# The order of the attention items on five engines: one schedule table for another

## The chip, the cores and the metric

The kernel runs on one core of a Trainium2 chip. The metric is the device time of one execution in microseconds. Each engine (TensorE, VectorE, ScalarE, GpSimd, and SyncE, which issues all DMAs) runs its own list of instructions in order; they meet only in semaphores.

## The reference

Three layers follow each other. The first is a gated linear attention with complex gates, over batch 4, 8 heads, sequence 768, head size 48:

```python
mag = np.sqrt(a_re * a_re + a_im * a_im)
scale = np.minimum(mag, 0.999) / (mag + 1e-06)
a_re_n, a_im_n = (a_re * scale, a_im * scale)
for t in range(S):
    new_re = ar * S_re - ai * S_im
    new_im = ar * S_im + ai * S_re
    S_re, S_im = (new_re + kv, new_im)      # kv: outer product of k[t] and v[t]
    y[:, :, t] = np.einsum('bhd,bhde->bhe', q[:, :, t], S_re)
```

Its output, as 3072 rows of 384, goes through two feed-forward layers: `elu(x @ w_in) @ w_out` with 2048 hidden columns, and `max(x @ w1, x @ w2, x @ w3) @ w_out` with 768. Everything is fp32.

## The kernel before

**Tiling.** The sequence is cut into 6 chunks of 128 steps. A unit is one chunk of two of the four batches, so there are 12 units (u) and 24 items (n = 2u and 2u+1, called "a" and "b" in the tables). Within a chunk the recurrence is done in parallel: log magnitude and angle of the gates are summed along time by scans, q and k are multiplied with the decays and rotated, sent through DRAM to be transposed, and then TensorE makes scores and outputs.

**The gate chain of a part** (part 0 and 1 are the two halves of unit 0, part p is unit p-1 from 2 on; a part has 384 columns in the first two and 768 after). ScalarE `square` (L709), GpSimd or VectorE `square_im`, VectorE `squared` (L968), ScalarE `root` (L716), VectorE `denominator` (L974) and `negative`, ScalarE `small` (L726, three operations) and `inverse` (L735, two), `tangent` on GpSimd (VectorE in the first two parts), ScalarE `arctan` (L742, with a table load before and after), VectorE `log_decay`, `signed`, `angle`, `scan_lam`, `center`, `scan_phi`, `reduced` (L984 to L1048), ScalarE `exps` (L751) and `end_gains` (called ends), GpSimd `decayed` (L607, twice), ScalarE `sines` (L767, with table loads), VectorE `rotate_q` and `rotate_k` (L1050, L1062).

**The items of a batch n.** SyncE `store_q`, `store_k`, then `load_qt`, `load_kt` bring the turned q and k back transposed. TensorE: `scores(n)` (here s(n), 16 matmuls from kt and qt), `k_rows(n)` (kr(n), 8 transposes), `outputs(n)` (y(n)), `increment(n)` (inc(n)). VectorE: `masked(n)` copies the scores out of PSUM under the mask, `state_decayed(n)` multiplies the state, `state_add(n)` adds the increment, `x_low(n)` makes the low part of the layer's output; ScalarE: `k_rows` and `x_high(n)`. These TensorE results live in a ring of 3 PSUM banks (L363 to L390); the order in which the banks are taken is the order of the table, and a bank is refilled only after its last reader.

**The first feed-forward layer** runs beside the attention, in 96 groups g. TensorE `first(g)` (L1310) and `second(g)` (L1329), two groups behind; ScalarE `exp_g` and `high_g` (expg, highg), VectorE `elu_g` (elu), GpSimd `low_g` (lowg). first(g) needs elu(g-2), second(g) needs lowg(g), expg(g) needs first(g) and lowg(g-2). first(0) needs the output of batch 1, first(8) that of batch 3, first(16) that of batch 7. fp32 products are made of three fp32r matmuls with high and low parts; the parts of the weights are made by `w_in_high`, `w_out_high` (ScalarE), `w_in_low` (VectorE), `w_out_low` (GpSimd, here wolow). The last layer runs alone on the engines from about 600 us.

**What sets the order.** Every item has a position x. For unit u it is 16u plus the entry of a table: AT_FIRST for u = 0 (AT_FIRST_B for part 1), AT_SECOND for u = 1, AT for the rest (L55 to L99). SPLIT (L100) holds the positions of the weights' loads and splits. Each engine's function `attention(x)` runs, for rising x, those items that have this x, in the fixed sequence of its own `if` lines (L507, L648, L847, L1145, L1350). Positions below START = 16 are run ahead of group 0; the others are spread between the halves of the groups by `after` (L337): one position per half group from g = 16 on. SyncE has no groups and only runs through x. So a table entry does nothing by itself: two items change places on an engine only if their entries cross.

Of the kernel before, what the change touches and what calls it, by code (L numbers as in the profile page):

```python
# [18 lines left out]
def build(nc, q, k, v, a_re, a_im, w_in, w_out, w1, w2, w3, w_fin, out):  # L19
# [46 lines left out]

    AT_FIRST = {
        "square": -49, "square_im": -49, "squared": -48, "root": -43, "denominator": -43, "inverse": -41, "log_decay": -39,
        "signed": -36, "tangent": -40, "arctan": -38, "angle": -35, "scan_lam": -39, "center": -38, "exps": -35, "ends": -28,
        "scan_phi": -35, "reduced": -34, "decayed_a": -33, "decayed_b": -32, "sines": -31, "rotate_q_a": -28, "rotate_k_a": -26,  # L70
        "rotate_q_b": -26, "rotate_k_b": -23, "state_decay": -13, "s_a": -5, "s_b": 1, "kr_a": -3, "kr_b": 2, "masked_a": -2,
        "masked_b": 2, "kr_evac_a": -1, "kr_evac_b": 3, "state_decayed_a": -22, "state_decayed_b": -12, "y_a": -1, "y_b": 3,
        "inc_a": 0, "inc_b": 3, "state_add_a": -1, "state_add_b": 6, "x_high_a": 0, "x_low_a": -1, "x_high_b": 4, "x_low_b": 6,
        "load_a": -50, "load_q": -48, "load_k": -44, "load_v": -44, "store_q_a": -27, "load_qt_a": -24, "store_k_a": -26,
        "load_kt_a": -24, "store_q_b": -24, "load_qt_b": -23, "store_k_b": -24, "load_kt_b": -20, "store_ends": -21,
        "load_ends": -12, "tile": -2, "negative": -41, "small": -41,
    }
# [7 lines left out]
    AT_SECOND = {
        "square": -40, "square_im": -38, "squared": -40, "root": -36, "denominator": -35, "inverse": -30, "log_decay": -29,
        "signed": -27, "tangent": -28, "arctan": -29, "angle": -23, "scan_lam": -28, "center": -24, "exps": -27, "ends": -28,
        "scan_phi": -22, "reduced": -18, "decayed_a": -28, "decayed_b": -27, "sines": -16, "rotate_q_a": -13, "rotate_k_a": -12,
        "rotate_q_b": -2, "rotate_k_b": -7, "state_decay": 8, "s_a": 1, "s_b": 6, "kr_a": 3, "kr_b": 10, "masked_a": 0,
        "masked_b": 7, "kr_evac_a": 2, "kr_evac_b": 8, "state_decayed_a": 5, "state_decayed_b": 5, "y_a": 3, "y_b": 10,  # L90
        "inc_a": 3, "inc_b": 11, "state_add_a": 3, "state_add_b": 11, "x_high_a": 3, "x_low_a": 3, "x_high_b": 11,
        "x_low_b": 11, "load_a": -62, "load_q": -60, "load_k": -59, "load_v": -2, "store_q_a": -15, "load_qt_a": -6,
        "store_k_a": -7, "load_kt_a": -5, "store_q_b": 1, "load_qt_b": 5, "store_k_b": 2, "load_kt_b": 5, "store_ends": -23,
        "load_ends": -19, "tile": 14, "negative": -34, "small": -30,
    }
# [1370 lines left out]
```

How the kernel before makes its waits and increments, by code:

```python
        def of_gate(eng, first, later, p):  # L306
            if p < PAIR:
                eng.wait_ge(first, p + 1)
            else:
                eng.wait_ge(later, p - 1)
# [1 line left out]
        def of_rows(eng, z):  # L312
            if z < 2 * PAIR:
                eng.wait_ge(qkd1, z + 1)
            else:
                eng.wait_ge(qkd, z - 2 * PAIR + 1)
# [1 line left out]
        def gates_loaded(eng, p):  # L319
            u = unit_of_part(p)
            if u == 0:
                eng.wait_ge(l_first[p], 32)
            else:
                eng.wait_ge(l_a[u % 2], 32 * ((u + 1) // 2))
# [52 lines left out]
        def filling(pe, what, n):  # L377
            z = place[what, n]
            if z >= RING:
                pe.wait_ge(free[z % RING], z // RING)
            return bank[ATT + z % RING], full[z % RING]
# [1 line left out]
        def filled(eng, what, n):  # L383
            z = place[what, n]
            eng.wait_ge(full[z % RING], z // RING + 1)
            return bank[ATT + z % RING], free[z % RING]
# [1 line left out]
        def emptied(eng, what, n):  # L388
            z = place[what, n]
            eng.wait_ge(free[z % RING], z // RING + 1)
# [36 lines left out]
            def load_a(p):  # L427
                u = unit_of_part(p)
                if users(p):
                    sp.wait_ge(phi0, users(p))
                if u == 0:
                    sp.dma_start(gates(p).ar, a_re[0, :, p:p + 1, :]).then_inc(l_first[p], 16)
                    sp.dma_start(gates(p).ai, a_im[0, :, p:p + 1, :]).then_inc(l_first[p], 16)
# [191 lines left out]
            def low_g(g):  # L625
                pool.wait_ge(ghi, g + 1)
                if g >= GR:
```

## Time and profile before

| | us |
|---|---|
| median of 3 runs | 900.1 |
| lowest and highest | 899.71 and 901.69 |
| the profiled execution | 900.1 |
| its span, first to last instruction | 898.3 |

| engine | busy us | share of the span | instructions |
|---|---|---|---|
| TensorE (PE) | 834.2 | 93% | 5584 |
| VectorE (DVE) | 425.3 | 47% | 628 |
| ScalarE (ACT) | 488.2 | 54% | 731 |
| GpSimd (POOL) | 318.1 | 35% | 254 |

The mean granted TensorE clock is 0.992 of full speed. The chain of work that ended last is 85% TensorE by the profile. The shares are means over stages; single stretches differ from them.

### The profile page before, as it was taken

Reading aid. Unit: us, or ns where it says so; the run is one execution under the profiler, and the core shown is the slowest. Engines: PE = TensorE matmul, PEld = TensorE weight load, DVE = VectorE, ACT = ScalarE, POOL = GpSimd, SP = SyncE. Lnnn points to the kernel's source line nnn. Section 1 sums busy time; section 2 is a strip of 40 time slices with the busy share of each in tenths; the row PEclk is TensorE's granted clock in tenths of the full one; section 3 lists DMA queues with packets and bytes.
Section 4 is the critical chain, followed back from the end, with each engine's and each line's share of the span. In section 5 each row is a group of like instructions: output and inputs, shape, how many; then the busy total and the mean of one; then the engine's idle time right before and its main releaser. Section 6 shows DMA issues by size and latency. Waiting matters only on the chain.

```text
span 898.3 us, 14185 instructions
## 1 busy us (share of the span) xinstructions
PE 834.2 (93%) x5584; PEld 712.9 (79%) x5584; DVE 425.3 (47%) x628; ACT 488.2 (54%) x731; POOL 318.1 (35%) x254
## 2 busy tenths in 40 slices
PE   0168989899999999999999999999999999999998
PEld 0158979888888888888888888888888888888886
DVE  6679795857475747574757422333112121202120
ACT  7778778586868686868686535643121121112111
POOL 1064643534343434343434323555122131313021
PEclk9998999999999999999999999999999999999999
DMA  7684353453435352534352533011010202000000
GB/s 301 167 220 127 94 177 92 144 159 111 140 93 161 108 144 90 165 104 134 100 168 66 161 119 147 0 49 75 13 59 0 71 1 71 0 36 1 24 13 35
DMA packets 70146, 88.43 MB, mean 98 GB/s; under 512 B 15296, under 2 KB 52672, under 8 KB 69568
## 3 DMA queue, kind: packets, MB, share of 16 engines
q1 hardware_dynamic: 70080, 87.53, 31.8%
q8 instruction: 44, 0.72, 0.4%
q14 instruction: 22, 0.18, 0.1%
HBM read 59.13 MB, written 28.39 MB: 97 GB/s over the span
## 4 chain that ended last, share of the span: by engine, by line
PE 85%; issue 4%; ACT 4%; POOL 3%; DVE 3%; DMA 1%; SPq 0%; DVEq 0%; ACTq 0%; POOLq 0%
PE bank L1243 83%; ACT t L704 2%; POOL gl L593 1%; PE bank L1258 1%; DMA ai<-in_a_im 1%; DVE t L944 1%; POOL wol L593 1%; POOL t L590 1%; DVE t L947 1%; DVE sc L947 0%; ACT L707 0%; ACT cs L704 0%; ACT woh L704 0%; ACT sn L704 0%; ACT xh L704 0%
## 5 line engine op out<-in xcount | busy, mean ns | idle before, releaser
L593 POOL TENSOR_TENSOR gl<-ge,gh 128x512 fp32r<-128x512 f32 x96 | 131.5, 1373 | 246.1 <-ACT gh L704 246.1
L947 DVE TENSOR_TENSOR hm<-bank,hm 128x512 f32<-128x512 f32 x72 | 49.8, 692 | 225.0 <-PE bank L1243 223.2
L1243 PE MATMUL bank<-gh,woh 128*128 128x512 f32 (+1 forms) x336 | 125.1, 372 | 1.2 <-POOL gl L593 1.2
L1243 PE MATMUL bank<-xh,wah 128*128 128x512 f32 x324 | 126.0, 389 | 0.0
L1243 PE MATMUL bank<-xl,wah 128*128 128x512 f32 x324 | 126.0, 389 | 0.0
L1243 PE MATMUL bank<-xh,wal 128*128 128x512 f32 x324 | 126.0, 389 | 0.0
L1243 PE MATMUL bank<-xh,wih 128*128 128x512 f32 (+1 forms) x336 | 123.5, 368 | 2.6 <-DVE ge L944 1.3
L1243 PE MATMUL bank<-xh,wil 128*128 128x512 f32 (+1 forms) x336 | 121.2, 361 | 0.0
L1243 PE MATMUL bank<-xl,wih 128*128 128x512 f32 (+1 forms) x336 | 121.1, 361 | 0.0
L1243 PE MATMUL bank<-gl,woh 128*128 128x512 f32 (+1 forms) x336 | 121.0, 360 | 0.0
L1243 PE MATMUL bank<-gh,wol 128*128 128x512 f32 (+1 forms) x336 | 120.9, 360 | 0.0
L593 POOL TENSOR_TENSOR hl<-hm,hh 128x512 fp32r<-128x512 f32 x36 | 46.5, 1292 | 204.3 <-ACT hh L704 204.3
L944 DVE SCALAR_TENSOR_TENSOR ge<-ge,bank 128x512 f32<-128x512 f32 x96 | 65.8, 686 | 104.8 <-ACT ge L704 104.0
L704 ACT ACTIVATE ge<-bank 128x512 f32<-128x512 f32 x96 | 57.0, 594 | 85.5 <-PE bank L1243 82.5
L704 ACT ACTIVATE t<-t 128x768 f32<-128x768 f32 (+1 forms) x117 | 91.8, 790 | 10.7 <-DVE t L947 3.2
L704 ACT ACTIVATE hh<-hm 128x512 fp32r<-128x512 f32 x36 | 22.7, 631 | 129.2 <-DVE hm L947 129.2
L1243 PE MATMUL bank<-qt,kt 96*128 96x128 f32 x384 | 50.5, 288 | 41.4 <-DMA kt<-k_cols 36.2
L704 ACT ACTIVATE gh<-ge 128x512 fp32r<-128x512 f32 x96 | 60.1, 626 | 43.0 <-DVE ge L944 23.2
L1243 PEld LDWEIGHTS bank<-qt,kt 96*128 96x128 f32 x384 | 49.3, 203 | 42.9 <-issue 41.7
L1243 PEld LDWEIGHTS bank<-gh,woh 128*128 128x128 f32 x336 | 63.7, 190 | 14.8 <-issue 4.5
L1243 PEld LDWEIGHTS bank<-xh,wih 128*128 128x128 f32 x336 | 64.1, 191 | 12.4 <-issue 2.1
L1243 PEld LDWEIGHTS bank<-xh,wil 128*128 128x128 f32 x336 | 64.0, 190 | 9.5
(86 smaller groups left out, 1524.5 us busy)
## 6 DMA issues: line engine op xcount, KB each, us to landing
q_cols<-qp SPq DMA_DIRECT2D x24, 384.0 KB, 2.8
k_cols<-kp SPq DMA_DIRECT2D x24, 384.0 KB, 3.5
qt<-q_cols SPq DMA_DIRECT2D x24, 384.0 KB, 4.2
kt<-k_cols SPq DMA_DIRECT2D x24, 384.0 KB, 3.7
vv<-in_v SPq DMA_DIRECT2D x12, 448.0 KB, 5.3
qd<-in_q SPq DMA_DIRECT2D x12, 384.0 KB, 5.1
kd<-in_k SPq DMA_DIRECT2D x12, 384.0 KB, 6.3
x_rows<-x2s SPq DMA_DIRECT2D x6, 768.0 KB, 5.4
```

What stands on the lines that cost most here:

```text
L590: return nc.gpsimd.tensor_tensor(dst, a, b, op)
L593: return nc.gpsimd.tensor_tensor(dst, whole, high.bitcast(f32), ALU.subtract)
L704: return nc.scalar.activation(dst, src, f, **kw)
L944: return nc.vector.scalar_tensor_tensor(out=dst, in0=a, scalar=s, in1=b, op0=op0, op1=op1)
L947: return nc.vector.tensor_tensor(dst, a, b, op)
L1243: return nc.tensor.matmul(dst, lhsT, rhs, start=start, stop=stop)
L1258: last = nc.tensor.transpose(dst[:, h * D2:(h + 1) * D2], kt[:, n % 2, HB * z + h, :], ident[0:D2, 0:D2])
```

## The change

Only the numbers in the five tables change, most by 1, a few by 2 to 5. No operation, tile or wait is added or taken away. The entries that change, as a diff:

```diff
     AT = {
-        "square": -21, "square_im": -23, "squared": -20, "root": -17, "denominator": -17, "inverse": -13, "log_decay": -14,
-        "signed": -9, "tangent": -11, "arctan": -10, "angle": -8, "scan_lam": -10, "center": -10, "exps": -7, "ends": -8,
-        "scan_phi": -8, "reduced": -6, "decayed_a": -8, "decayed_b": -8, "sines": -4, "rotate_q_a": -4, "rotate_k_a": -2,
-        "rotate_q_b": 1, "rotate_k_b": 4, "state_decay": 2, "s_a": 6, "s_b": 10, "kr_a": 7, "kr_b": 11, "masked_a": 5,
-        "masked_b": 10, "kr_evac_a": 7, "kr_evac_b": 11, "state_decayed_a": 6, "state_decayed_b": 6, "y_a": 7, "y_b": 11,
-        "inc_a": 9, "inc_b": 15, "state_add_a": 9, "state_add_b": 15, "x_high_a": 8, "x_low_a": 8, "x_high_b": 12,
+        "square": -21, "square_im": -22, "squared": -20, "root": -17, "denominator": -17, "inverse": -13, "log_decay": -13,
+        "signed": -8, "tangent": -11, "arctan": -10, "angle": -8, "scan_lam": -10, "center": -10, "exps": -7, "ends": -8,
+        "scan_phi": -7, "reduced": -6, "decayed_a": -9, "decayed_b": -8, "sines": -4, "rotate_q_a": -4, "rotate_k_a": -2,
+        "rotate_q_b": 1, "rotate_k_b": 5, "state_decay": 3, "s_a": 6, "s_b": 10, "kr_a": 7, "kr_b": 11, "masked_a": 6,
+        "masked_b": 10, "kr_evac_a": 7, "kr_evac_b": 11, "state_decayed_a": 6, "state_decayed_b": 8, "y_a": 8, "y_b": 11,
+        "inc_a": 10, "inc_b": 15, "state_add_a": 10, "state_add_b": 15, "x_high_a": 9, "x_low_a": 9, "x_high_b": 12,
...
-        "store_k_a": -2, "load_kt_a": 2, "store_q_b": 2, "load_qt_b": 8, "store_k_b": 8, "load_kt_b": 9, "store_ends": -6,
+        "store_k_a": -2, "load_kt_a": 6, "store_q_b": 6, "load_qt_b": 8, "store_k_b": 8, "load_kt_b": 8, "store_ends": -6,
...
     SPLIT = {
-        "w_in_high": (-9, 8, 9, 20), "w_out_high": (-10, 6, 16, 25), "w_in_low": (0, 14, 16, 27), "w_out_low": (-5, 2, 13, 32),
-        "w_load": (-44, -43, -20, -4),
+        "w_in_high": (-4, 9, 11, 20), "w_out_high": (-10, 8, 16, 25), "w_in_low": (1, 14, 16, 27), "w_out_low": (-6, 2, 13, 28),
+        "w_load": (-44, -43, -20, -8),
```

In AT_FIRST, AT_FIRST_B and AT_SECOND some 45 entries change likewise. Crossings of two items by engine, all that there are of weight:

- SyncE, prologue: load_v(0) ahead of load_a(2); load_q(1), load_k(1) behind w_load(0), w_load(1); store_q(1) ahead of load_qt(0); w_load(3) ahead of store_ends(1); load_kt(2) ahead of load_qt(2). Every later unit: load_kt(2u+1) ahead of the next load_q and load_k. Every second unit: store_x2 ahead of load_kt(2u) (was behind store_q(2u+1)).
- TensorE: kr(3) ahead of second(1). Every unit from u = 2: y(2u) behind the next second (but y(4) keeps its place); s(2u+1) ahead of inc(2u), which then stands right behind it.
- ScalarE: root(0) ahead of square(1), inverse(1) ahead of small(1), small(2) ahead of inverse(2), exps(2) ahead of ends(2), square(3) ahead of w_in_high(2). Every unit: x_high(2u) behind the next expg (in unit 3 only behind ends).
- VectorE: tangent(1) ahead of scan_lam(0), center(1) behind signed(1) and angle(0), reduced(0) behind scan_phi(1), squared(2) behind rotate_k(1), log_decay(3) behind state_add(2), signed(3) behind elu(3), state_add(3) behind w_in_low(3). Every unit: rotate_k(2u+1) and masked(2u) behind an elu in front of which one or both stood, state_decayed(2u+1) behind center, state_add(2u) behind masked(2u+1), x_low(2u) and scan_phi behind an elu.
- GpSimd: w_out_low(3) ahead of lowg(5). Every unit: a lowg behind the first decayed instead of ahead of it, square_im behind the next lowg.

## Rows read from the trace of the kernel before

**Rows 1.** Busy time by stretch: us, busy us (x instructions) per engine, clock, DMA share, GB/s.

```profile
62.00:80.00 18.00, 12.23 (x109) 11.71 (x108) 15.47 (x14) 14.46 (x20) 11.09 (x4) 0.81 0.80 248
...
140.00:180.00 40.00, 36.35 (x400) 35.25 (x398) 29.81 (x42) 30.60 (x45) 17.41 (x14) 0.96 0.45 131
180.00:225.00 45.00, 45.00 (x370) 39.15 (x371) 28.05 (x44) 34.38 (x53) 17.97 (x16) 1.00 0.44 134
...
800.00:898.30 98.30, 95.17 (x420) 78.45 (x418) 16.21 (x25) 18.14 (x30) 19.18 (x15) 1.00 0.06 22
...
163.00:166.00 3.00, 3.00 (x65) 2.62 (x58) 2.93 (x5) 2.94 (x5) 0.00 (x0) 0.61 0.88 290
```

**Rows 2.** TensorE's timeline, 60 to 185 us: start, us, operation, idle before it.

```profile
61.79 0.36 PE L1243 MATMUL bank<-xh,wih 128*128 128x256 f32 x1
...
68.78 3.75 PE L1243 MATMUL bank<-qt,kt 96*128 96x128 f32 x16 [4.60 <-issue]
...
82.21 1.95 PE L1243 MATMUL bank<-qt,kt 96*128 96x128 f32 x16
...
101.48 0.38 PE L1243 MATMUL bank<-gh,woh 128*128 128x256 f32 x1 [1.15 <-POOL gl L593]
...
108.04 0.28 PE L1243 MATMUL bank<-xh,wih 128*128 128x256 f32 x1
...
113.82 0.36 PE L1243 MATMUL bank<-xh,wih 128*128 128x256 f32 x1 [1.30 <-DVE ge L944]
...
123.23 0.43 PE L1243 MATMUL bank<-sc,vv 128*32 128x128 f32 x8 [2.27 <-DVE st L947]
...
134.80 0.43 PE L1243 MATMUL bank<-sc,vv 128*32 128x128 f32 x8 [0.25 <-DVE sc L947]
...
162.82 0.42 PE L1243 MATMUL bank<-sc,vv 128*32 128x128 f32 x8 [1.76 <-issue]
...
179.99 0.50 PE L1243 MATMUL bank<-xh,wih 128*128 128x512 f32 x1 [1.27 <-DVE xl L947]
```

**Rows 3.** Timeline of ScalarE and VectorE in the prologue.

```profile
6.28 0.52 ACT L704 ACTIVATE t<-ar 128x384 f32<-128x384 f32 x1 [1.99 <-DMA ai<-in_a_im]
...
25.66 0.56 DVE L947 TENSOR_TENSOR t<-t 128x384 f32<-128x384 f32 x1
...
34.83 4.20 ACT L704 ACTIVATE t<-t 128x768 f32<-128x768 f32 x5 [1.03 <-DVE t L947]
...
46.57 1.26 DVE L947 TENSOR_TENSOR sc<-bank,mask 128x512 f32<-128x512 f32 x2
```

**Rows 4.** Timelines of ScalarE, GpSimd and VectorE, 90 to 125 us.

```profile
91.00 0.87 ACT L704 ACTIVATE kr<-bank 128x384 f32<-128x384 f32 x2 [1.23 <-PE bank L1258]
...
98.64 2.78 POOL L593 TENSOR_TENSOR gl<-ge,gh 128x512 fp32r<-128x512 f32 x1
...
108.75 3.52 POOL L593 TENSOR_TENSOR wol<-wor,woh 128x1536 fp32r<-128x1536 f32 x1
...
109.80 3.28 DVE L947 TENSOR_TENSOR t<-t 128x768 f32<-128x768 f32 x1 [2.17 <-ACT t L704]
...
121.30 2.36 DVE L947 TENSOR_TENSOR st<-st,decay 96x192 f32<-96x192 f32 x4
```

**Rows 5.** Timelines of one steady unit, 280 to 311 us.

```profile
280.69 1.07 ACT L704 ACTIVATE x2s<-bank 128x512 f32<-128x512 f32 x2
...
280.01 0.33 SPq L479 DMA_DIRECT2D kt<-k_cols  x1
...
280.30 0.96 DVE L947 TENSOR_TENSOR t<-t 128x768 f32<-128x768 f32 x1 [1.19 <-ACT t L704]
...
291.74 1.95 PE L1243 MATMUL bank<-qt,kt 96*128 96x128 f32 x16
...
310.53 0.43 PE L1243 MATMUL bank<-sc,vv 128*32 128x128 f32 x8
...
305.46 1.01 POOL L590 TENSOR_TENSOR qd<-qd,cs 128x384 f32<-128x384 f32 x1 [4.40 <-ACT sn L704]
```

More of the change, by code:

```diff
@@ L67, in build @@
     AT_FIRST = {
[L68 to L76, printed above, removed]
+        "square": -49, "square_im": -49, "squared": -48, "root": -46, "denominator": -44, "inverse": -42, "log_decay": -39,
@@ new lines, in build @@
+        "signed": -36, "tangent": -40, "arctan": -38, "angle": -34, "scan_lam": -38, "center": -37, "exps": -34, "ends": -28,
+        "scan_phi": -34, "reduced": -33, "decayed_a": -33, "decayed_b": -32, "sines": -31, "rotate_q_a": -28, "rotate_k_a": -26,
+        "rotate_q_b": -26, "rotate_k_b": -24, "state_decay": -13, "s_a": -6, "s_b": 2, "kr_a": -3, "kr_b": 5, "masked_a": -2,
+        "masked_b": 2, "kr_evac_a": -1, "kr_evac_b": 3, "state_decayed_a": -20, "state_decayed_b": -12, "y_a": -2, "y_b": 5,
@@ L77, in build @@
+        "inc_a": 0, "inc_b": 5, "state_add_a": -1, "state_add_b": 6, "x_high_a": 0, "x_low_a": -1, "x_high_b": 4, "x_low_b": 6,
+        "load_a": -50, "load_q": -48, "load_k": -45, "load_v": -46, "store_q_a": -27, "load_qt_a": -24, "store_k_a": -27,
+        "load_kt_a": -24, "store_q_b": -25, "load_qt_b": -23, "store_k_b": -24, "load_kt_b": -20, "store_ends": -22,
+        "load_ends": -12, "tile": -2, "negative": -43, "small": -41,
     }
     AT_FIRST_B = {
-        "square": -43, "square_im": -45, "squared": -45, "root": -42, "denominator": -40, "inverse": -38, "log_decay": -36,
@@ L81, in build @@
-        "signed": -34, "tangent": -38, "arctan": -36, "angle": -33, "scan_lam": -36, "center": -36, "exps": -31, "ends": -27,
-        "scan_phi": -33, "reduced": -29, "sines": -29, "load_a": -49, "negative": -40, "small": -40,
+        "square": -45, "square_im": -45, "squared": -45, "root": -44, "denominator": -40, "inverse": -40, "log_decay": -36,
+        "signed": -35, "tangent": -38, "arctan": -36, "angle": -33, "scan_lam": -36, "center": -34, "exps": -32, "ends": -27,
+        "scan_phi": -33, "reduced": -29, "sines": -30, "load_a": -49, "negative": -40, "small": -38,
@@ L83, in build @@
     }
     AT_SECOND = {
-        "square": -40, "square_im": -38, "squared": -40, "root": -36, "denominator": -35, "inverse": -30, "log_decay": -29,
-        "signed": -27, "tangent": -28, "arctan": -29, "angle": -23, "scan_lam": -28, "center": -24, "exps": -27, "ends": -28,
+        "square": -39, "square_im": -37, "squared": -39, "root": -35, "denominator": -34, "inverse": -30, "log_decay": -31,
+        "signed": -27, "tangent": -28, "arctan": -29, "angle": -22, "scan_lam": -28, "center": -24, "exps": -27, "ends": -26,
@@ L88, in build @@
         "scan_phi": -22, "reduced": -18, "decayed_a": -28, "decayed_b": -27, "sines": -16, "rotate_q_a": -13, "rotate_k_a": -12,
[L89 to L92, printed above, removed]
@@ L93, in build @@
-        "store_k_a": -7, "load_kt_a": -5, "store_q_b": 1, "load_qt_b": 5, "store_k_b": 2, "load_kt_b": 5, "store_ends": -23,
-        "load_ends": -19, "tile": 14, "negative": -34, "small": -30,
+        "rotate_q_b": -2, "rotate_k_b": -7, "state_decay": 8, "s_a": 1, "s_b": 6, "kr_a": 3, "kr_b": 8, "masked_a": 0,
+        "masked_b": 7, "kr_evac_a": 3, "kr_evac_b": 8, "state_decayed_a": 5, "state_decayed_b": 5, "y_a": 3, "y_b": 10,
+        "inc_a": 3, "inc_b": 11, "state_add_a": 3, "state_add_b": 12, "x_high_a": 3, "x_low_a": 3, "x_high_b": 11,
@@ L95, in build @@
+        "x_low_b": 11, "load_a": -61, "load_q": -59, "load_k": -58, "load_v": -2, "store_q_a": -15, "load_qt_a": -3,
+        "store_k_a": -9, "load_kt_a": -5, "store_q_b": 1, "load_qt_b": 5, "store_k_b": 2, "load_kt_b": 5, "store_ends": -23,
+        "load_ends": -19, "tile": 14, "negative": -33, "small": -34,
     }
```

## The prediction

> **What bounds the kernel now.** I read the busy time by stretch first, then TensorE's own timeline, then the other engines around each hole in it. From 180 us on TensorE has work in every microsecond (45.00 of 45) until the last product; after that 3.13 us of evacuation and store close the span [rows 1]. Its matmuls are not changed, so a gain there is impossible and only a new wait can move that part. What can move lies ahead of 180 us: the gate chain of the prologue, after which first(0) starts at 61.79, and the holes behind it. They are 5.77 us between 62 and 80 and 3.65 between 140 and 180 [rows 1], and one by one 4.60 ahead of s(2), 1.15 ahead of second(3), 1.30 ahead of first(8), 2.27 ahead of y(4), 0.25 (after 0.29 and 0.30 at kr(5)) ahead of y(5), 1.76 ahead of y(6) and 1.27 ahead of first(16) [rows 2]. I take these as checkpoints: start of an item before, start after, difference. The profiled execution took 900.1 us with a span of 898.3; 900.1 is also the median of the three runs, so no correction is needed.
>
> **The change part by part.** No instruction is added or removed. A position only matters where it alters the order of two items on one engine, since each engine runs in order and waits on semaphores. TensorE's order up to first(0) is the same, and so is all after the last attention unit. I follow the new orders, each item starting when its engine is free and its last input is there.
>
> *Prologue, -0.7.* ScalarE idled 1.99 us for the second gate load until 6.28 and only then ran square(1), root(0), root(1) [rows 3]. Now root(0) stands ahead of square(1): its three operations of 0.5 us run from 5.0, square(1) from 6.5, root(1) ends at 9.1 instead of 9.57, and what follows on ScalarE moves with it. On VectorE center(1) now fills a 0.2 us gap ahead of scan_phi(0), so the last subtraction of reduced(1), which ended at 26.22 [rows 3], ends at 25.5. Everything up to masked(0) (46.57 [rows 3]) hangs on it. In part 2 small goes ahead of inverse: log_decay and scan_lam come earlier, tangent and arctan later by small's three operations (2.5 us of the 4.20 of five [rows 3]), and signed(2) needs both: even, by my count (0.3 us either way). first(0) at 61.1. The V load put ahead of the unit-1 gates delays those by about 1.5 us, and they aren't used until 29.5: nothing.
>
> *s(2), nothing.* It waits for kt(2) and qt(2), which share the queue with 768 KB of gates. The two loads swap places; the same bytes land before s(2). The 4.60 us and the slow clock after it (s(2) took 3.4 us start to start against 1.7 for s(3) [rows 2]) stay.
>
> *kr(3) ahead of second(1), -1.2.* The evacuation of kr(3) waited 1.23 us for TensorE at 91.00 [rows 4]; kr(3) is now 2.2 us earlier. exps(3) follows at 90.5, decayed(4) and (5) end at 96.7, lowg(3) at about 98.5 instead of 101.42 (98.64 plus 2.78 [rows 4]). second(3) no longer waits: 99.6 for 101.48, -1.9 so far.
>
> *Given back at first(7), +0.95.* signed(3) now stands behind elu(3), so the angle, and load_a(4) behind it, come 0.2 us later; ScalarE's square(4), the table load and sines(3) keep their places, and expg(5) starts at 104.9. first(7) needs elu(5). It waits until 107.1; it started at 108.04 [rows 2]: -0.95.
>
> *wolow(3) moved ahead of lowg(5), -0.75.* It ran 3.52 us from 108.75, and denominator(4) on VectorE took 3.28 us beside it, against 0.96 of a later one of its kind [rows 4, 5]. Now it runs from 101.0 to 104.5, in a gap of GpSimd, beside rotate_q(4). denominator(4) is short, small(4) 2 us earlier, elu(6) ends at 112.1, and so starts first(8) (113.82 [rows 2]): -1.7. What it runs beside matters: the Trainium skill (SBUF — State Buffer, "Who interferes with whom") says that a VectorE instruction with two SBUF inputs and a GpSimd one that reads SBUF exclude each other for the whole instruction. denominator(4) ended 0.8 us after wolow(3), as by that rule. By it rotate_q(4) waits out wolow(3) and costs the 0.3 us that make elu(5) end at 107.1; if they only shared, 106.8 and 0.3 us more gain, no more.
>
> *y(4), a wait that moves.* VectorE's state_decayed took 2.36 us beside GpSimd's tangent(4) [rows 4]. masked(4) now stands behind elu(8), and elu(8) behind expg(8), which ScalarE reaches at 118.1 after small, inverse and highg(7). masked(4) ends at 121.25, state_decayed(4) at 121.85: y(4) at 121.9 for 123.23, -1.35. kr(4) waits in front of it for the same mask.
>
> *s(5) ahead of inc(4).* The ring of three PSUM banks now makes y(5) wait for state_add(4), which stands behind scan_phi(4) and masked(5) on VectorE: 132.65 for 134.80 [rows 2], -2.15.
>
> *y(6) behind second(12).* The 2.2 us of second(12) cover state_decayed(6), so the wait of 1.76 goes: y(6) at 160.95 for 162.82. Behind the hole the clock fell (mean 0.96 in 140 to 180 [rows 1]); y(6) and second(12) took 5.7 us where the same work takes 4.2. Without the hole I count 1.5 us for that too. But then the other engines are late: inc(6) waits 1.05 us for x_low(6) (it needs y(6)'s bank), y(7) 1.7 us for state_add(6), which needs expg(15), elu(15) and masked(7), and first(16) for x_low(7): 176.0 for 179.99 [rows 2]. **-4.0** in all.
>
> *Steady part, nothing.* Per unit of 44.8 us: lowg now stands behind one decayed, which started at 305.46 [rows 5]; it is done 3 us before its second. store_x2 goes ahead of kt(12), which was issued at 280.01 while x2s was written at 280.69 to 281.76 [rows 5]. kt then goes out at 282.4 and, behind 768 KB, lands by 289 (1152 KB at the 248 GB/s of 62 to 80 us [rows 1] are 4.8 us; 2 us are for the start); s(12) starts at 291.74 [rows 5]. load_q and load_k behind kt(13) land at 304, with decayed at 305.5. y(13), at 310.53 [rows 5], now needs state_add(12), done at 308.6: 1.9 us to spare. If this cover goes, each us late costs one us in each of six units.
>
> Sum: -0.7 (first(0)), -1.2 (second(3)), +0.95 (first(7)), -0.75 (first(8)), +0.35 (y(4)), -0.8 (y(5)), -1.85 (first(16)): -4.0. Span 894.3, time **896.1**.
>
> **The rivals.**
> 1. *A new wait in every unit (slower).* Place: y of each odd batch, for state_add of the even one. For it: the chain elu, x_low, scan_phi, mask, add is now in one line on VectorE, and an operation of 0.96 us has been seen to take 3.28 [rows 4]. Against: that was beside a 3.52 us GpSimd operation, of which the steady part has none. It decides beyond 1.9 us late; at 2.9 us late it costs 6 x 1.0, so -4 + 6 = +2: 902.1.
> 2. *The start keeps its pace (the change does little).* ScalarE's sines, small and inverse, not the moved items, set when elu comes; every hole closed opens again at the next elu, as at first(7). Only 0.7 us of the prologue and 0.5 remain: 898.9. For it: my own count gives back 0.95 there. Against: denominator(4) was on that chain.
> 3. *All new waits vanish.* From s(6) at 154.05 there are 19.25 us of work to first(16): 173.3, -6.7, time 893.4. It needs x_low and state_add 2.7 us earlier than I find.
> 4. *The slow clock stays.* TensorE stood for 1.76 us and ran part of y(6) at the lower level (1.2 GHz of 2.4; the mean is 0.61 in 163 to 166 [rows 1]). New holes of about 1 us at kr(4), inc(6) and y(7) might bring it too: -4.0 + 1.5 = -2.5, time 897.6. The Trainium skill (TensorE: Matmul & The Clock Gate, "Part 1: The HAM clock gate") has the clock follow recent activity, seen through a free-running window, so that it varies by run; no run here shows the variation.
>
> **How the numbers follow.** Forecast 0.45 (own range 894.5 to 897.3), rival 1 0.15, rival 2 0.15, rival 3 0.15, rival 4 0.10. Eight in ten reach from rival 3, with a little more for a better prologue, to between rivals 2 and 1: 892.5 to 901. A difference of 0.2% is 1.8 us: faster than 898.3 are the forecast, rivals 3 and 4 and a bit of 2, less a tenth for my chain of small steps, 0.67; rival 2 and the mild part of 1 are within, 0.18; slower 0.15.
>
> **What would show it.** first(0) near 61.1 (right if 60.7 to 61.5); no idle ahead of second(3); elu(5) the releaser of first(7); denominator(4) near 1 us; y(6) without idle and no clock below full at 160 to 166; first(16) at about 176; TensorE busy 45 of 45 from 180 on. Wrong it is if first(16) comes after 178.5, or if any stretch after 180 shows a hole that repeats by unit, ahead of y or s.

## Result and profile after

The change made the kernel slower: 907.9 us (median of 6 timed runs, 905.2 to 909.3) against 901.1 (899.7 to 902.1) beside it; the ratio of the means, over all 31 executions of the changed kernel on record, is 1.0065 [1.0051, 1.008]. Forecast were 896.1, range 892.5 to 901.0. The profiled execution after took 907.6 us with a span of 905.8, so 7.5 us of span are to be found.

Busy time by stretch of the changed kernel (us, busy us (x instructions) of TensorE, weight loads, VectorE, ScalarE, GpSimd, clock, DMA share, GB/s):

```profile
120.00:130.00 10.00, 7.48 (x98) 6.76 (x97) 9.93 (x16) 6.97 (x11) 5.38 (x3) 0.83 0.63 190
140.00:180.00 40.00, 37.07 (x397) 36.00 (x399) 28.95 (x43) 30.76 (x46) 19.20 (x14) 1.00 0.44 131
163.00:166.00 3.00, 3.00 (x35) 2.87 (x37) 2.97 (x5) 0.00 (x0) 3.00 (x2) 1.00 0.46 133
180.00:225.00 45.00, 42.33 (x322) 36.40 (x312) 28.11 (x43) 31.87 (x47) 15.86 (x14) 0.96 0.46 134
184.00:188.00 4.00, 4.00 (x15) 3.24 (x14) 1.03 (x3) 3.91 (x5) 0.41 (x1) 0.60 0.00 0
225.00:315.00 90.00, 89.59 (x703) 75.46 (x702) 60.17 (x88) 68.52 (x102) 39.13 (x33) 1.00 0.42 125
800.00:905.80 105.80, 102.65 (x453) 84.65 (x451) 16.22 (x25) 19.33 (x32) 19.19 (x15) 1.00 0.06 23
```

Beside [rows 1]: the tail after the last product is 3.15 us (3.13 before), and the slow stretch at 163 to 166 is gone; but 180 to 225 is no longer full (42.33 of 45), there is a slow stretch at 184 to 188 (the clock was 1.00 there before), another in 120 to 130 (1.00 before), and 225 to 315 has small holes where TensorE had none (90.00 of 90). TensorE's timeline after, the rows that answer to [rows 2], and two new ones at 124 and 174:

```profile
68.92 3.78 PE L1243 MATMUL bank<-qt,kt 96*128 96x128 f32 x16 [4.75 <-DMA qt<-q_cols]
...
100.66 0.39 PE L1243 MATMUL bank<-gh,woh 128*128 128x256 f32 x1
...
110.50 0.39 PE L1243 MATMUL bank<-xh,wih 128*128 128x256 f32 x1 [3.11 <-DVE ge L944]
115.53 0.35 PE L1243 MATMUL bank<-xh,wih 128*128 128x256 f32 x1 [0.46 <-DVE ge L944]
124.16 0.55 PE L1258 MATMUL bank<-ident,kt 96*128 96x96 f32 x4 [1.89 <-DVE sc L947]
125.34 0.42 PE L1243 MATMUL bank<-sc,vv 128*32 128x128 f32 x8 [0.63 <-DVE st L947]
137.37 0.43 PE L1243 MATMUL bank<-sc,vv 128*32 128x128 f32 x8 [0.18 <-DVEq L1095]
165.79 0.43 PE L1243 MATMUL bank<-sc,vv 128*32 128x128 f32 x8
174.36 0.85 PE L1243 MATMUL bank<-vv,kr 128*96 128x64 f32 x8 [1.39 <-DVE xl L947]
183.60 0.64 PE L1243 MATMUL bank<-xh,wih 128*128 128x512 f32 x1 [2.67 <-DVE xl L947]
275.64 0.50 PE L1243 MATMUL bank<-xh,wih 128*128 128x512 f32 x1 [0.35 <-DVE xl L947]
```

They are s(2), second(3), first(7), first(8), kr(4)'s second half, y(4), y(5), y(6), inc(6), first(16) and first(32). As checkpoints (start after less start before, forecast beside it):

| | s(2) | second(3) | first(7) | first(8) | y(4) | y(5) | y(6) | first(16) | end |
|---|---|---|---|---|---|---|---|---|---|
| measured | +0.1 | -0.8 | +2.5 | +1.7 | +2.1 | +2.6 | +3.0 | +3.6 | +7.5 |
| forecast | 0 | -1.9 | -0.95 | -1.7 | -1.35 | -2.15 | -1.9 | -4.0 | -4.0 |

Until second(3) it is ahead of before. The loss comes at first(7), in small steps from there to first(16), and behind first(16).

**First(7).** VectorE and GpSimd of the changed kernel around 105 us: rotate_q(4), signed's last step, elu(5), later denominator(4); and lowg and wolow(3) on GpSimd.

```profile
103.77 1.46 DVE L947 TENSOR_TENSOR qp<-qd,cs 128x384 f32<-128x384 f32 x1 [1.01 <-ACT cs L704]
105.14 3.84 DVE L947 TENSOR_TENSOR qp<-qd,sn 128x384 f32<-128x384 f32 x1
108.91 0.94 DVE L944 SCALAR_TENSOR_TENSOR t<-t 128x768 f32<-128x768 f32 x1
109.77 0.67 DVE L944 SCALAR_TENSOR_TENSOR ge<-ge,bank 128x512 f32<-128x512 f32 x1
...
113.55 0.96 DVE L947 TENSOR_TENSOR t<-t 128x768 f32<-128x768 f32 x1 [2.17 <-ACT t L704]
```

```profile
103.51 1.29 POOL L593 TENSOR_TENSOR gl<-ge,gh 128x512 fp32r<-128x512 f32 x1
104.77 3.79 POOL L593 TENSOR_TENSOR wol<-wor,woh 128x1536 fp32r<-128x1536 f32 x1
```

A product of 128x384 that takes 0.55 us alone takes 3.84: it starts 0.37 us after wolow(3) and ends 0.42 after it. denominator(4), which no longer stands beside wolow(3), is at 0.96 for 3.28 [rows 4]. By the rule of the Trainium skill that the prediction weighed (SBUF — State Buffer, "Who interferes with whom") this is what happens to two SBUF inputs beside a GpSimd read; the trace agrees.

**Between y(6) and first(16).** GpSimd, VectorE and ScalarE of the changed kernel: tangent(5); scan_lam(5), the copy behind it and, later, the subtraction of reduced(5); arctan(5), square(6) and x_high(7).

```profile
163.07 3.91 POOL L590 TENSOR_TENSOR t<-ai,t 128x768 f32<-128x768 f32 x1
```

```profile
163.61 1.75 DVE L1017 TENSOR_TENSOR_SCAN t<-restart,t 128x768 f32<-128x768 f32 x1
165.39 1.62 DVE L1025 COPY ends<-t 128x12 f32<-128x12 f32 x1
...
179.93 1.64 DVE L947 TENSOR_TENSOR t<-t 128x768 f32<-128x768 f32 x1
```

```profile
167.01 0.84 ACT L704 ACTIVATE t<-t 128x768 f32<-128x768 f32 x1 [4.03 <-POOL t L590]
...
181.66 0.84 ACT L704 ACTIVATE t<-ar 128x768 f32<-128x768 f32 x1 [2.31 <-DVE t L947]
182.41 0.47 ACT L704 ACTIVATE xh<-bank 128x384 fp32r<-128x384 f32 x1
```

The tangent took 2.02 us before. Now it lasts until 1.6 us behind the end of the scan, and the copy of 128x12, 0.17 us alone, lasts until the tangent is done. ScalarE waits 4.03 us for it (2.12 before). Behind that come the evacuation of kr(6), for which s(7) has a hole of 0.84 us, and elu and x_low(6), for which inc(6) has one of 1.39. Later the subtraction takes 1.64 us for 0.96 beside decayed; ScalarE's square waits for it, and x_high(7), in line behind the square, starts 1.5 us after y(7) has ended. So the hole ahead of first(16) is 2.67 us for 1.27 before.

**The steady part.** VectorE in one steady unit, first of the kernel before (rows not shown so far), then after. They are the three instructions of reduced(7) and elu(31):

```profile
263.63 1.28 DVE L941 TENSOR_SCALAR t<-t 128x768 f32<-128x768 f32 x1
264.95 0.96 DVE L947 TENSOR_TENSOR t<-t 128x768 f32<-128x768 f32 x1
265.94 0.17 DVE L1048 COPY last_turn<-t 128x6 f32<-128x6 f32 x1
266.39 0.69 DVE L944 SCALAR_TENSOR_TENSOR ge<-ge,bank 128x512 f32<-128x512 f32 x1 [0.27 <-ACT ge L704]
```

```profile
269.14 1.60 DVE L941 TENSOR_SCALAR t<-t 128x768 f32<-128x768 f32 x1
270.77 1.64 DVE L947 TENSOR_TENSOR t<-t 128x768 f32<-128x768 f32 x1
272.45 0.86 DVE L1048 COPY last_turn<-t 128x6 f32<-128x6 f32 x1
273.22 0.67 DVE L944 SCALAR_TENSOR_TENSOR ge<-ge,bank 128x512 f32<-128x512 f32 x1
```

and GpSimd after, in the same stretch:

```profile
269.02 1.30 POOL L593 TENSOR_TENSOR gl<-ge,gh 128x512 fp32r<-128x512 f32 x1
270.27 1.33 POOL L590 TENSOR_TENSOR qd<-qd,cs 128x384 f32<-128x384 f32 x1
271.56 1.72 POOL L590 TENSOR_TENSOR kd<-kd,sn 128x384 f32<-128x384 f32 x1
273.24 1.30 POOL L593 TENSOR_TENSOR gl<-ge,gh 128x512 fp32r<-128x512 f32 x1
```

Read the two together: 269.14 waits for lowg (until 270.3), the product of qd for 269.14's last part, 270.77 for that product (until 271.6), kd's product for 270.77 (until 272.4), and the copy of 128x6, 0.17 us of work, for kd's product (until 273.28). Each waits for the one under way on the other engine. elu(31) waited 0.27 us for ScalarE before; now it stands behind VectorE's own queue and is late, so x_low(11) is, and first(32), which needs the whole of it, waits 0.35 us. first(48) waits 0.34 us in the same way; no later first of a layer tile does.

### The profile page after: what moved, and what is told of

It is laid out like the page before. It is cut to its first block, busy times and chain, and to the rows that moved or that the text cites. A ratio compares the mean times of both kernels' runs of the same rounds, so it can differ in the third digit from the quotient of the medians.

```text
span 905.8 us, 14185 instructions
## 1 busy us (share of the span) xinstructions
PE 840.5 (93%) x5584; PEld 715.7 (79%) x5584; DVE 443.3 (49%) x628; ACT 489.2 (54%) x731; POOL 335.1 (37%) x254
## 4 chain that ended last, share of the span: by engine, by line
PE 59%; issue 0%; ACT 0%; DVE 0%
PE bank L1243 59%; PE bank L1258 0%; ACT osb L704 0%; DVE xl L947 0%
## 5 line engine op out<-in xcount | busy, mean ns | idle before, releaser
L1243 PE MATMUL bank<-xh,wih 128*128 128x512 f32 (+1 forms) x336 | 125.7, 374 | 6.9 <-DVE ge L944 3.6
L1243 PE MATMUL bank<-qt,kt 96*128 96x128 f32 x384 | 52.4, 295 | 41.9 <-DMA kt<-k_cols 35.7
```

Of the source, the lines that this page charges most:

```text
L1243: return nc.tensor.matmul(dst, lhsT, rhs, start=start, stop=stop)
```

## Experiments

Measured times are medians; the ratio is to the kernel before on the same chip. One kernel's runs lie up to 6 us apart, so I also compare checkpoints. "Steady" below is the time from second(14) to the last second product, second(95), in the profiled execution, behind all that happens at the start: 416.87 us before, 419.20 after. The whole loss of 7.5 us is thus 3.6 at first(16), 1.6 of low clock from there to second(14) (+5.2), and 2.3 steady.

**e1: wolow(3) back.** In SPLIT `"w_out_low": (-6, 2, 13, 28)` to `(-6, 2, 13, 32)`.

> The changed kernel with one entry put back: w_out_low's last position is 32 again, so wolow(3) stands behind lowg(5) on GpSimd. Theory (exclusion): in the changed kernel rotate_q(4) on VectorE took 5.29 us because its second half stood out the whole of wolow(3), elu(5) came 3.76 us late and first(7) waited 3.11 us. Put back, rotate_q(4) takes about 1.6 us, TensorE has no hole of more than 0.3 us ahead of first(7), and the 3.3 us denominator(4) returns with a hole of about 1.3 us ahead of first(8). TensorE reaches first(16) 1.5 to 2.5 us earlier than in the changed kernel (183.6): time about 905.5 to 906 against 907.9. Rival (it is the new order behind y(4)): that delays first(16) by itself, so first(16) stays within 0.7 us of 183.6 and the time at 907.5 to 908.

Measured 907.65 (903.5 to 909.6), ratio 1.0072 [1.0052, 1.0092]; profiled run 903.8. rotate_q(4) 2.00 us, first(7) 106.82 without a wait, denominator(4) 3.25 again, first(16) 181.30. In the profile 2.3 us come back at first(16), and no low clock stands behind it (one stood in 172 to 177, mean 0.66); of the median nothing. So exclusion makes the wait at first(7); that the whole gets faster without it is not shown, since nine executions of e1 lie 6 us apart.

**e2: inverse ahead of small.** In AT_SECOND `"small": -34` to `-30`.

> The changed kernel with inverse(2) ahead of small(2) again (small at -30 in the second table). Theory: the 0.76 us that the prologue gains by root(0) ahead of square(1) is lost because tangent(2) on GpSimd now runs beside scan_lam(2) and takes 2.7 us instead of 1.8, and small's 2.5 us delay the arctan. Put back, signed(2) starts at 41.0 instead of 41.95, masked(0) at about 45.8, first(0) at 60.8 to 61.1 instead of 61.79, and the whole ends about 0.9 us earlier: about 907.0. Rival: first(0) hangs on the banks and on w_in_low(0), not on the gate chain; first(0) stays within 0.2 us and so does the time (907.9).

906.52, ratio 1.0065 [1.0042, 1.0089]. signed(2) at 41.08 for 41.95, first(0) 59.56, second(3) 99.44 for 100.66. first(7) is at 109.28 and first(16) at 182.39: 1.2 us of the gain reach there, 1.3 the end. first(0) gained 2.2 us, more than the 0.7 to 1.0 expected; signed(2) accounts for 0.9 of it, and y(1) took 1.08 us where in the changed kernel it took 1.94: in e2 TensorE had its full clock there already.

**e3: decayed back.** In AT `"decayed_a": -9` to `-8`.

> The changed kernel with decayed_a at -8 again from unit 2 on: a lowg stands ahead of both decayed of a unit, not between them. Theory: the lowg between them pushes decayed(odd) to where VectorE has reduced, which takes 4.1 us instead of 2.4; elu, highg and x_high behind it come late, and first(32) and first(48) wait 0.35 us each, 0.75 us lost for each layer tile. Put back, reduced(7) takes under 3 us, no hole of over 0.1 us stands ahead of first(32) or first(48), and the time is 1.5 to 2.5 us less: about 906. Rival: the late start of reduced (state_add and masked now stand ahead of it) is the cause; reduced(7) still ends behind 272.5 relative to first(31) at 268.1 and the holes stay: 907.9.

907.87, ratio 1.0081 [1.0057, 1.0106]; steady 419.00. reduced(7) stays at 4.09 us. lowg no longer stands between the two decayed; now it stands behind them, and the copy of reduced(7) waits for it (1.14 us). The theory that its place alone makes the collision is refuted.

**e4: the steady table back.** All of AT as before; AT_FIRST, AT_FIRST_B, AT_SECOND and SPLIT of the change.

> The changed kernel with the whole table for units 2 to 11 put back to the one before; the tables for units 0 and 1 and the weights' positions stay new. Theory: units 2 to 11 cost what is lost behind y(4): the holes ahead of s(7), inc(6) and first(16), the slow clock behind first(16), and 0.75 us for each of three layer tiles; the loss at first(7) (2.45 us against before) stays. Time 902 to 904.5; first(26) to the end as long as before within 0.2 us. Rival: the loss at first(7) passes through to the end whatever the later order, and 905.5 or more remain.

901.57, under the range expected, ratio 1.0008 [0.9994, 1.0022]; steady 416.88. first(7) still waits until 109.85, but first(16) comes at 180.86. So of the 7.5 us of span 6.6 (by the medians, each against the kernel before beside it, 5.4 of 6.8) are in the table of units 2 and later, part of it felt already in their first batches, and half of the 1.8 us lost at first(7) is paid back by first(8) and y(4) (1.1 and 0.8 us late), since denominator(4) takes 0.96 us.

**e5: e4 and e1 together.**

> The changed kernel with the steady table of before and, besides, the last position of wolow(3) back at 32. Theory A (wolow(3) beside rotate_q(4) is the whole of the wait at first(7), and that wait counts): rotate_q(4) near 1.6 to 2.0 us, elu(5) near 106.0, first(7) at 106.8 or 106.9 without a wait, first(16) about 179, time 899 (2 us under the kernel with only the steady table back, 901.6; 1 us under before). Rival B (the wait at first(7) is paid back by later slack, because denominator(4) takes its 3.28 us again and y(4) waits on the mask): first(7) early, but first(16) at 180.5 to 181 and the time 901 to 901.6, as before.

900.9, ratio 1.0001 [0.999, 1.0011]: no difference. One of the 12 executions took 1081.8 us, at a mean clock of 0.756; the ratio leaves it out. The profiled run (898.5) follows theory A, with first(7) at 106.68 and first(16) at 178.39; the median doesn't.

**e6, e7, e8: the steady positions in three groups, each alone on the kernel before.**

```
e6  y_a 8, inc_a 10, state_add_a 10, masked_a 6, x_high_a 9, x_low_a 9
e7  log_decay -13, signed -8, scan_phi -7
e8  square_im -22, state_decay 3, decayed_a -9, rotate_k_b 5, state_decayed_b 8,
    load_kt_a 6, store_q_b 6, load_kt_b 8
```

> The kernel before with six steady positions of the change alone: y_a 8, inc_a 10, state_add_a 10, masked_a 6, x_high_a 9 and x_low_a 9, so s of the odd batch ahead of inc of the even one, y behind one more down product, and the even batch's evacuations later. Theory A (these pack x_low, scan_phi, masked and state_add ahead of reduced on VectorE and put x_high ahead of exps on ScalarE, so reduced meets decayed on GpSimd): a hole ahead of first(32), first(48) and on, 0.4 to 0.7 us per layer tile, reduced(7) 3.5 us or more against 2.41, time 904 to 906. Rival B (the gate chain's own moves, signed, scan_phi and log_decay, make it late): no hole in the steady part, first(32) to end as before, time 899 to 901.

> The kernel before with three steady positions of the change alone: log_decay -13, signed -8 and scan_phi -7. Theory A (the order of TensorE and its evacuations makes the loss): the steady part as before, time 899.5 to 901. Rival B (signed behind an elu makes angle, scan_phi and reduced later by the wait for it): reduced(7) starts 1 us later and meets the first half of nothing new but pushes elu(31), holes ahead of first(32) and on, time 904 to 906.

> The kernel before with the other steady positions of the change alone: square_im -22, state_decay 3, decayed_a -9, rotate_k_b 5, state_decayed_b 8, load_kt_a 6, store_q_b 6, load_kt_b 8, thus GpSimd's, the queue's and two of VectorE's. Theory A: no steady loss, time 899.5 to 901.5. Rival C (lowg between the two decayed puts the second one beside reduced, with no help from the others): reduced(7) over 3 us, holes ahead of first(32) and on, 903 to 906.

e6 904.6, ratio 1.0049 [1.0032, 1.0066]; e7 903.14, 1.0037 [1.0024, 1.0049]; e8 903.58, 1.0035 [1.0022, 1.0047]. Each costs 3 to 4 us, but steady they take 417.34, 416.84 and 417.40: little or nothing. Their loss lies ahead of first(16) (4.4, 3.1 and 4.6 us there). I had expected it behind, in e6 alone; that e6's time fell into theory A's range is luck. e6 is only 0.5 us late at y(6) and loses all the rest in one place, TensorE first, then VectorE (angle(5), scan_phi(5), x_low(6)):

```profile
173.92 1.33 PE L1243 MATMUL bank<-vv,kr 128*96 128x64 f32 x7 [4.45 <-DVE xl L947]
```

```profile
167.97 1.93 DVE L944 SCALAR_TENSOR_TENSOR t<-t,ar 128x768 f32<-128x768 f32 x1
169.93 0.85 DVE L947 TENSOR_TENSOR t<-t,last_turn 128x6 f32<-128x6 f32 x1
170.81 2.51 DVE L1036 TENSOR_TENSOR_SCAN t<-restart,t 128x768 f32<-128x768 f32 x1
173.25 0.53 DVE L947 TENSOR_TENSOR xl<-bank,xh 128x384 fp32r<-128x384 f32 x1
```

y(6) behind second(12) has no hole any more, and s(7) starts 4.5 us earlier than before (1.3 of them because inc(6) now stands behind it). But x_low(6), at 167.94 before, now stands behind scan_phi(5) and comes at 173.25; inc(6) waits 4.45 us for it and then runs at half clock:

```profile
174.00:178.00 4.00, 4.00 (x23) 4.00 (x24) 2.69 (x5) 0.63 (x1) 1.08 (x2) 0.50 0.02 1
```

In the changed kernel x_low(6) starts at 173.66, ahead of scan_phi(5) at 174.13, so this wait is e6's and not that of the whole change. e8 loses 1.4 us at y(4): masked(4) stands ahead of rotate_k(5) there, whose two products meet lowg and tangent(4) and take 1.58 and 2.15 us for 0.55 each.

**e9: decayed cut to 8 columns.** In decayed, for units from 2 on, `[:, e, :]` to `[:, e, 0:8]` in the changed kernel.

> The changed kernel with GpSimd's two products of decayed cut from 384 columns to 8 in units 2 and later (so q and k of these units keep their values undecayed beyond column 8; everything else is done). In the changed kernel reduced(7) takes 4.10 us on VectorE where its three instructions take 1.68 at best, and the copy of 128x6 alone 0.86 for 0.17. Theory A (VectorE and GpSimd instructions with SBUF operands wait each other out, one by one, and that is what makes elu(31) and first(32) late): reduced(7) 1.7 to 1.9 us, no hole ahead of first(32) and first(48), from first(16) to the last second() 419.0 to 419.6 us against 422.96, time 902.5 to 905. Rival B (the order on VectorE and ScalarE makes it late, whatever GpSimd does): the holes stay, 422 us or more, time 906 or more.

900.6 (one run; 2 us less than theory A's lower end), steady 417.35, and 419.53 from first(16) on, as theory A had it. The same three instructions and elu(31):

```profile
263.94 1.53 DVE L942 TENSOR_SCALAR t<-t 128x768 f32<-128x768 f32 x1
265.51 0.96 DVE L948 TENSOR_TENSOR t<-t 128x768 f32<-128x768 f32 x1
266.50 0.17 DVE L1049 COPY last_turn<-t 128x6 f32<-128x6 f32 x1
266.58 0.68 DVE L945 SCALAR_TENSOR_TENSOR ge<-ge,bank 128x512 f32<-128x512 f32 x1
```

Only the first still waits, for a lowg. 2.66 us, not the 1.9 expected, but the repeated hole is gone with VectorE's and ScalarE's order unchanged: the repeated hole is GpSimd's doing. Of the 2.3 us of steady loss 1.85 are gone; the 0.5 that are left are the same as in e6 (417.34). first(16) comes at 179.98, as before; part of that is from the start, since decayed(4) is cut too and wolow(3) is done early (first(7) 107.20).

**e10: w_out_low in four.** In the changed kernel, one instruction of 128x1536 (1792 in the expectation is a slip) becomes four of 128x384:

```
-low(wol[:, cols, :], wor[:, cols, :], woh[:, cols, :]).then_inc(wolo, 1)
+for c in range(4 * z, 4 * z + 4):
+    last = low(wol[:, c, :], wor[:, c, :], woh[:, c, :])
+last.then_inc(wolo, 1)
```

> The changed kernel with each w_out_low, one GpSimd instruction of 128x1792 elements, written as four of a quarter each, at the same place. Theory A (each pair of instructions excludes, so a VectorE instruction waits for at most the GpSimd instruction that is under way): rotate_q(4), 5.29 us as two instructions of 0.55 beside one of 3.8, falls to 2.2 to 3.6 us; elu(5) ends 1.7 to 3 us earlier, first(7) at 107.5 to 109. Rival B (the two share SBUF bandwidth for as long as GpSimd has work, so cutting it changes nothing): rotate_q(4) 4.8 us or more, first(7) at 110.5. Little of it reaches the end by either.

907.06 (one run). rotate_q(4), VectorE, and wolow(3), GpSimd:

```profile
105.36 1.47 DVE L949 TENSOR_TENSOR qp<-qd,cs 128x384 f32<-128x384 f32 x1 [1.00 <-ACT cs L706]
106.75 1.37 DVE L949 TENSOR_TENSOR qp<-qd,sn 128x384 f32<-128x384 f32 x1
```

```profile
106.37 5.58 POOL L593 TENSOR_TENSOR wol<-wor,woh 128x384 fp32r<-128x384 f32 x4
```

2.84 us for 5.29, inside A's 2.2 to 3.6: the wait is for one instruction, not for as long as GpSimd has work. elu(5) and first(7) (110.47, as rival B had it, against theory A's 107.5 to 109) gained nothing, because this run was 1.6 us late at second(3).

**e11: AT_FIRST and AT_FIRST_B of the change alone.**

> The kernel before with AT_FIRST and AT_FIRST_B of the change alone (the gate chain of the first unit and its evacuations; second and steady tables and SPLIT as before). Theory A (they bring 0.7 us at first(0) where small and inverse keep their order, and the holes behind, set by ScalarE and VectorE of later units, keep their distance): root(2) 0.7 us earlier, first(0) at 61.0 to 61.3, the end 0.3 to 0.8 us earlier, time 899.3 to 900. Rival B (a hole of part 2 eats it, as in the changed kernel): first(0) 61.6 or later, 900 to 901.5. Rival C (s(2) waits for its loads to 68.8 whatever comes before, so nothing of it reaches the end): first(0) early, s(2) at 68.7 to 68.9, time 900 to 900.6.

899.09, ratio 0.9988 [0.9976, 1.0]. signed(2) 40.98 for 41.73, first(0) 60.73, first(16) 178.74. A little better, at the edge of what can be told.

**e12: e5 with inverse ahead of small.** `"small": -30`.

> The steady table of before, the first and second tables of the change but inverse ahead of small again (small -30), and the last wolow at 32. Theory A (the parts add: first(0) 2.2 us early as with inverse ahead, first(7) without wait, no loss behind): first(16) 177.5 to 178.5, time 897.5 to 899.5, faster than before by 0.1 to 0.25%. Rival B (s(2)'s loads and VectorE's masks give the fixed points, and the gain is lost at each): first(16) 178.4 to 180.5, time 899.5 to 901.

898.85 (12 runs), ratio 0.9985 [0.9974, 0.9996]; first(16) 177.62. Faster than before, as theory A had it. But first(0) came at 61.05, only 0.7 us early where 2.2 were expected: the mean clock in 58 to 65 us was 0.52, where e2 had 1.00 in 57 to 65.

**e13, e14, e15: pairs of the groups (e6+e7, e6+e8, e7+e8), and e16: e12 with w_out_low in four.**

> The kernel before with the ring positions (y_a, inc_a, masked_a, state_add_a, x_high_a, x_low_a) and the gate positions (log_decay, signed, scan_phi) of the change. Theory A (the hole needs exps late, by x_high ahead of it, and reduced close behind it, so that both decayed meet it): reduced(7) 3.3 us or more, first(16) to the last second product 421 to 423 us against 419.05 before. Rival B (it needs lowg between the two decayed, which only the third group brings): reduced(7) under 3.3, 419.0 to 419.6.

> The kernel before with the ring positions and the third group (square_im, state_decay, decayed_a, rotate_k_b, state_decayed_b, loads and stores) of the change. Theory A of e13 (signed behind elu isn't needed for reduced to meet decayed): reduced(7) 3 us or more, 420 to 423 us from first(16) to the last second product. Rival B: under 419.8, since without the gate moves VectorE has its slack ahead of reduced.

> The kernel before with the gate positions and the third group of the change, TensorE's order as before. Theory A (x_high ahead of exps and the packed evacuations are needed): reduced(7) 3.1 to 3.5 us, but elu(31) still inside its slack: no hole, 419.0 to 419.7 us from first(16) to the last second product. Rival B (GpSimd beside reduced is enough by itself): 421 us or more.

> The kernel of e12 with each w_out_low, one GpSimd instruction of 128x1792 elements, written as four of a quarter each. In e12 wolow(3) runs beside denominator(4), which takes 3.3 us for 0.96, and small(4), elu(6), first(8) hang on that. Theory A (VectorE waits only for the GpSimd instruction under way): denominator(4) 1.3 to 2 us, first(8) 0.8 to 1.7 us earlier than in e12 (112.32), y(4) and y(6) keep part of it, the end 0.3 to 1.2 us earlier, time 897.5 to 898.7. Rival B (the mask and state_decayed set y(4) whatever first(8) does, so nothing reaches the end): 898.7 to 899.5.

Steady, second(14) to second(95), with reduced(7):

| | before | e6 | e7 | e8 | e13 | e14 | e15 | after | e9 |
|---|---|---|---|---|---|---|---|---|---|
| steady, us | 416.87 | 417.34 | 416.84 | 417.40 | 417.43 | 417.58 | 419.29 | 419.20 | 417.35 |
| reduced(7), us | 2.41 | 2.44 | 3.33 | 3.10 | 3.11 | 3.41 | 3.60 | 4.10 | 2.66 |

e15, without any move on TensorE, loses as much in the steady part as the whole change, in somewhat other places: 0.15 us of idle ahead of first(32), first(48) and first(64) each and 0.24 ahead of y(20) and y(22). Rival B was right there, and my theory, that x_high ahead of exps and the packed evacuations are needed, fell; so it did in e13 and e14, whose 419.60 and 419.74 us from first(16) on are under its 420. The gate positions and the third group are each harmless or nearly so (reduced(7) of 3.33 and 3.10 us ends inside the slack) and together are not. Which position of the third group it takes is open: by e3 it isn't decayed_a alone. Times of one run each: 901.29, 904.73, 905.87. At the start the losses do not add: e13, with the moves of e6 and of e7, is 0.6 us late at first(16), where these two alone are 4.4 and 3.1. tangent(5) takes 3.90 to 3.92 us in every kernel that has both the ring positions and the third group (after, e1, e2, e3, e9, e10, e14) and 2.0 to 2.1 in every other one.

e16: 896.54 (6 runs, 895.6 to 898.2), ratio 0.9958 [0.9944, 0.9972], 1 us better than theory A's lower end. denominator(4), VectorE, and wolow(3), GpSimd:

```profile
107.45 1.76 DVE L949 TENSOR_TENSOR t<-t 128x768 f32<-128x768 f32 x1 [2.17 <-ACT t L706]
```

```profile
106.41 4.97 POOL L593 TENSOR_TENSOR wol<-wor,woh 128x384 fp32r<-128x384 f32 x4
```

1.76 us for 3.28. first(8) at 109.96, y(4) 119.37, first(16) 175.24, 2.4 us ahead of e12 (0.85 of it stood ahead of first(7) already).

**e17: the kernel before with w_out_low in four, nothing else.**

> The kernel before with nothing changed but each w_out_low written as four instructions of a quarter (128x384) each. Theory A (the cut itself is worth what e16 gained over e12, 896.54 against 898.85): denominator(4) 1.7 to 1.9 us for 3.28, first(8) 1 to 1.8 us earlier than 113.82, y(4), y(6) and first(16) with it, time 898 to 899. Rival B (it works only with the start of e12): 900 to 901.

898.97 (11 runs), ratio 0.9983 [0.9973, 0.9993], and denominator(4) 1.76: theory A. first(8) 111.98 for 113.82, of which 0.4 stand ahead of first(7) already, first(16) 177.38 for 179.98. The cut and e12's start add up to e16 (0.9983 x 0.9985 = 0.9968, in e16's interval), the best version here.

## Why the prediction was wrong

At the end the sum had -4.0 us and the trace has +7.5. Of these 11.5 us, 1.1 are there at second(3), 2.3 come at first(7), 1.3 at y(5), 2.9 between y(5) and first(16), and 3.9 behind it, where the sum had nothing. **The step that failed** is the same in most of them: for a moved item the prediction asked who needs its result, and put at nothing what it runs beside on VectorE or GpSimd. It priced a new neighbour only for wolow(3), and there at the wrong time. Term by term:

**Prologue, -0.7: right for ScalarE, wrong behind it.** Square(1) and root went as worked out; reduced(1)'s subtraction stands at 24.91 for 25.66 [rows 3], square(2) starts at 28.75 for 29.50. Then small ahead of inverse was called even, within 0.3. It cost about 0.9 (e2: signed(2) 41.08 for 41.95): tangent(2) takes 2.69 us on GpSimd beside a scan on VectorE, where it took 1.81. first(0) stood at 61.79, as before.

**s(2), nothing:** right (68.92).

**kr(3) ahead of second(1), -1.2:** the order was right, the size not: second(3) -0.8 in place of -1.9, without its idle time, as forecast. lowg(3), forecast to end at 98.5, ended at 100.6, because decayed(4), 2.7 us before and 3.7 after, met scan_phi(3) and reduced(3).

**wolow(3) moved, -0.75: the first large step that failed.** I let it run from 101.0 to 104.5, and by the skill's rule priced the collision at 0.3 us. GpSimd was late (square_im(4) took 2.98 us beside w_in_low(3), 1.46 before), wolow(3) ran from 104.77 to 108.56 and caught the second half of rotate_q(4). The rule was right and was used; its price hung on a start 3.8 us off. The collision was moved from denominator(4) (2.3 us) to rotate_q(4) (3.7), ahead of an earlier elu. In the sum this falls on the term of first(7), +0.95 by forecast and +3.3 by the trace; the term of first(8) itself came out, -0.75.

**y(4), +0.35: right.** From first(8) to y(4) the difference grew by 0.4; the wait moved to kr(4), 1.89 us, as forecast. **y(5), -0.8: wrong**, +0.5: behind the holes at kr(4) and y(4) the clock fell (mean 0.83 in 120 to 130), which I had not counted.

**y(6) behind second(12), -1.85: the wait at y(6) went, those behind it were mis-sized.** y(6) has no idle and 163 to 166 is at full clock, as forecast. From y(6) to first(16) the sum had 15.05 us; it took 17.81. The holes are 0.84 at s(7) (forecast none), 1.39 at inc(6) (1.05), 0.13 at y(7) (1.7) and 2.67 at first(16), 5.0 in all; beside the 12.8 us of work the sum had room for 2.3, less than the 1.05 and 1.7 that it names. What was left out is what runs beside: tangent(5), 3.91 us for 2.02, which makes the arctan and all in line behind it late, and reduced(5), which makes x_high(7) late. With decayed cut (e9) the hole at first(16) is 1.27 again; what tangent(5) costs is read from the trace alone, no run took it away by itself. e6, that group alone, waits 4.45 us at inc(6) in another way: x_low(6) stands behind angle(5)'s last steps and scan_phi(5), which took 1.93, 0.85 and 2.51 us beside lowg and decayed where they take 0.96, 0.17 and 1.76 alone. The kernel before has them drawn out already (1.24, 0.85 and 2.52 us), so that was to be read beforehand. The end of this stretch was -4.0 by my sum, +3.6 by the trace: 4.8 of these 7.6 us were there at y(6).

**Steady part, nothing: wrong, by the term that I left out.** I wrote that lowg, now behind one decayed, "is done 3 us before its second", and so checked who needs its result. The result was not late; reduced, on the other engine, was, because lowg and the second decayed now ran beside it. Rival 1 named an operation drawn out as its ground and ruled it out: the steady part "has none" as long as 3.52 us. Pieces of 1.0 to 1.3 us do it too, since VectorE's three instructions each catch one. Its place was wrong as well (first of a layer tile, not y), the size small: 2.3 us in all, 1.85 of them by the collision (e9). The queue was right: s(12) and y(13) do not wait.

**The slow clock (rival 4):** it left 163 to 166 and came back at 125 to 129, and at first(16), where a hole of 2.67 us stood ahead (0.60 in 184 to 188), 1.6 us. The Trainium skill (TensorE: Matmul & The Clock Gate, "Part 1: The HAM clock gate") says that how much of a kernel's start runs at the lower clock varies from run to run of the same kernel. The traces agree: the changed kernel and e3 have the same order up to decayed(4) at 93 us, and in 61 to 65 us a mean clock of 1.00 and 0.50. That the clock makes the spread of the times isn't shown: executions of the changed kernel with the same mean clock, 0.991, took from 904.9 to 909.3 us.

Open: why e1's median shows nothing of its profile's gain; what spreads the times of one kernel; what e7 and the rest of e8 lose ahead of first(16), where holes and low clock mix; and why the groups' losses there do not add.

## What to carry to other kernels

Before moving an instruction in an order written by hand, lay VectorE's and GpSimd's timelines side by side: an item that is late for nobody can still stop the other engine, and the short critical item beside it pays. Cut long GpSimd instructions that stand beside VectorE's chain; in this kernel that alone gave 0.17%, and 0.42% with the better start. When a wait is cured on TensorE, ask at once what the next item waits for in the evacuating engine's queue: in e6 some 3 us gained by s(7) were all given back there.
